# The hand-written order of work between the dense layer and the routed experts is rearranged on all five engines

## The reference

```
h = x @ w_in
g = h where h >= 1, 0 where h <= -1, (h + 1)^2 / 4 between
x = g @ w_out
```

```
logits = x @ w_gate;  e = argmax(logits);  p = softmax(logits)[e]
out[token] = p * (relu(x[token] @ w1[e]) @ w2[e])
```

## Time and profile before

| | |
|---|---|
| median of 3 runs | 822.27 us |
| the profiled execution | 820.93 us |
| its span, first to last instruction | 819.0 us |
| TensorE busy | 763.2 us, 93% |
| VectorE busy | 593.1 us, 72% |
| ScalarE busy | 423.7 us, 52% |
| mean granted TensorE clock | 0.991 |

### The profile page before, as it was taken

The page is one execution under the profiler, slowest core; times in us unless marked ns, Lnnn a source line. Parts: engine busy times, 40 slices in busy tenths (PEclk is TensorE's granted clock), DMA queues, the critical chain, the costliest instruction groups (busy, mean ns, idle before and its releaser), DMA issues. The chain is left out here.

```text
span 819.0 us, 17200 instructions
## 1 busy us (share of the span) xinstructions
PE 763.2 (93%) x5765; PEld 741.7 (91%) x5765; DVE 593.1 (72%) x1006; ACT 423.7 (52%) x649; POOL 319.0 (39%) x297
## 2 busy tenths in 40 slices
PE   2788999999999999999999999979859999999994
PEld 1788999999999999999999999979859999999994
DVE  4653868787878787878878788568667676867850
ACT  3023445454545454545454555655466676767751
POOL 2442544534343445454444544540633323232111
PEclk9999999999999999999999999999988999999998
DMA  6962222222222223232333200542987535545300
GB/s 202 313 168 75 77 92 76 91 75 91 75 91 75 92 81 93 81 96 87 94 86 98 86 24 1 177 123 65 297 303 243 186 108 193 165 153 169 114 21 5
DMA packets 41457, 97.05 MB, mean 119 GB/s; under 512 B 6935, under 2 KB 24481, under 8 KB 39754
## 3 DMA queue, kind: packets, MB, share of 16 engines
q1 hardware_dynamic: 37498, 87.46, 33.7%
q0 software_dynamic: 3920, 9.08, 4.1%
HBM read 105.63 MB, written 9.33 MB: 140 GB/s over the span
## 5 line engine op out<-in xcount | busy, mean ns | idle before, releaser
L545 POOL TENSOR_TENSOR g_t<-u_t,r_t 128x512 f32<-128x512 f32 x96 | 135.8, 1415 | 255.5 <-ACT u_t L695 255.4
L690 ACT ACTIVATE r_t<-bank,neg 128x512 f32<-128x512 f32 x96 | 66.0, 687 | 186.8 <-PE bank L1384 186.8
L1396 PE MATMUL bank<-wo_h,g_h 128*128 128x328 f32 x384 | 127.3, 332 | 2.1 <-DVE g_l L1006 2.1
L1000 DVE TENSOR_SCALAR u_t<-bank 128x512 f32<-128x512 f32 x96 | 66.0, 688 | 75.6 <-ACT r_t L690 52.0
L1396 PE MATMUL bank<-wo_h,g_l 128*128 128x328 f32 x384 | 120.1, 313 | 0.0
L1396 PE MATMUL bank<-wo_l,g_h 128*128 128x328 f32 x384 | 120.1, 313 | 0.0
L627 POOL DMA_INDIRECT out_x<-ob,idx_tok x31 | 38.2, 1234 | 155.0 <-ACT ob L765 150.7
L695 ACT ACTIVATE u_t<-u_t,half 128x512 f32<-128x512 f32 x96 | 69.4, 723 | 40.9 <-DVE u_t L1000 39.7
L936 DVE TENSOR_TENSOR_SCAN W<-W,cst 128x512 f32<-128x512 f32 x48 | 83.4, 1740 | 4.9 <-DMA W<-decays 4.9
L1517 PE MATMUL bank<-w_h,h_h 128*128 128x320 f32 x248 | 78.4, 316 | 2.6 <-DVE w_l L1061 1.5
L1384 PE MATMUL bank<-xT_h,wi_h 128*128 (+1 forms) x384 | 78.8, 287 | 1.6 <-issue 1.6
(11 more groups left out here) (231 smaller groups left out, 1953.3 us busy)
## 6 DMA issues: line engine op xcount, KB each, us to landing
raw<-in_w SPq DMA_DIRECT2D x12, 1280.0 KB
W<-decays SPq DMA_DIRECT2D x24, 512.0 KB, 5.1
raw<-in_w SPq DMA_DIRECT2D x12, 1024.0 KB
raw2n<-in_w SPq DMA_DIRECT2D x7, 1280.0 KB
raw1n<-in_w SPq DMA_DIRECT2D x7, 1024.0 KB
raw<-in_w SPq DMA_DIRECT2D x24, 256.0 KB
qG<-in_q SPq DMA_DIRECT2D x24, 180.0 KB
qT<-in_qt SPq DMA_DIRECT2D x48, 80.0 KB
```

The lines of the kernel that those rows point to most:

```text
L545: pool.tensor_tensor(g_t[p % 2][:, :], u_t[p % 2][:, :], r_t[p % 2][:, :], ALU.add).then_inc(sm["g_done"], 1)
L690: act.activation(r_t[p % 2][:, :], bank_h[p % 2][:, :], ACT.Relu, bias=neg1[:, 0:1]).then_inc(sm["r_done"], 1)
L1000: dve.tensor_scalar(u_t[p % 2][:, :], bank_h[p % 2][:, :], 1.0, -1.0, ALU.min, ALU.max).then_inc(sm["u_done"], 1)
L1396: mm = pe.matmul(bank_acc[tt][:, 0:DL], l[p % 4][:, c], r[:, f, :], start=f == 0 and a == 0, stop=f == NT1 - 1 and a == 2)
```

## The change

No arithmetic is changed. What is changed is order:

- TensorE: `second2(0)` is cut in two, tiles 0 to 3 before `first_wide(1, ...)` and tiles 4 to 7 behind `turn_y(2)` and `turn_experts(2)`. `second2(1)` moves behind `first_wide(2, ...)`, `second2(2)` behind `first2(3)` and `turn_y(4)`, and the loop begins at slot 3.
- ScalarE: `w1_high(1)` and `w1_high(2)` move ahead, `out_gate(0)`, `w2_high(0, 1)`, `w2_high(1)` and `w2_high(2)` move back.
- VectorE: the same for the low parts, and `w2_low(0, 1)` moves behind the operation that writes `rowi`. `w1_low(0)` goes one step later in the last block and `w2_low(0, 0)` goes into `tail`.
- SyncE: `refill(1)` goes ahead of `refill2(0)`; `refill2(1)` goes behind `load_routed2(3)`; from slot 3 on `refill(s)` and `refill2(s - 1)` take turns.
- GpSimd: `gather(2)` moves from `tail` into step 6 of the last block.

```diff
             def last_stores(t):
                 store_x2(t)
+                refill(1)
                 refill2(0)
-                refill(1)
...
             sp.wait_ge(sm["e_listed"], 2)
             load_routed(3)
-            refill2(1)
             refill(2)
             load_routed2(3)
-            refill(3)
-            refill(4)
-            refill2(2)
-            refill2(3)
-            for s in range(5, NS):
+            refill2(1)
+            for s in range(3, NS):
                 refill(s)
                 refill2(s - 1)
...
-                    if not att and p in (4, 5):
+                    if not att and p in (4, 5, 6):
                         gather(p - 4)
...
             h_high(0, 0)
             h_high(0, 1)
-            w2_high(0, 1)
+            w1_high(1, 0)
             h_high(0, 2)
-            w1_high(1, 0)
+            w1_high(1, 1)
             h_high(0, 3)
             y_high(1)
-            w1_high(1, 1)
+            w2_high(0, 1)
+            h_high(1, 0)
+            h_high(1, 1)
+            h_high(1, 2)
+            h_high(1, 3)
+            w1_high(2, 0)
+            y_high(2)
+            w1_high(2, 1)
             act.wait_ge(sm["list_done"], 1)
             out_gate(0)
-            h_high(1, 0)
+            h_high(2, 0)
             w2_high(1, 0)
-            h_high(1, 1)
+            h_high(2, 1)
             w2_high(1, 1)
...
+            h_high(2, 2)
+            h_high(2, 3)
+            w1_high(3, 0)
+            w1_high(3, 1)
+            y_high(3)
             out_gate(1)
-            h_high(2, 0)
...
             w2_high(2, 0)
-            h_high(2, 3)
             w2_high(2, 1)
-            y_high(3)
             w1_high(4, 0)
...
+                        if p in (6, 7):
+                            w1_low(0, p - 6)
 
             def tail(t):
+                w2_low(0, 0)
                 g_low(t, NP1 - 1)
...
             dve.tensor_copy(rowi[:, :], row[:, :]).then_inc(sm["row_ready"], 1)
-            h_low(1, 3)
+            w2_low(0, 1)
+            y_low(2)
+            w1_low(2, 0)
             dve.wait_ge(sm["tab_T"], 3)
...
             dve.tensor_tensor(e_new[:, EARLY:NS], ...).then_inc(sm["e_listed"], 1)
+            w1_low(2, 1)
+            h_low(2, 0)
+            w2_low(1, 0)
+            h_low(2, 1)
             w2_low(1, 1)
-            y_low(2)
-            w1_low(2, 0)
-            w1_low(2, 1)
+            h_low(2, 2)
             dve.wait_ge(sm["tab_T"], 4)
...
                 turn_y(1)
-                second2(0)
+                second2(0, range(0, NT2 // 2))
                 for p in range(4):
                     first_wide(1, p)
+                turn_y(2)
                 turn_experts(2, bank_r[:, 256:384], HALVES)
-                turn_y(2)
-                second2(1)
+                second2(0, range(NT2 // 2, NT2))
+                for p in range(3):
+                    first_wide(2, p)
                 turn_table(2, bank_r[:, 0:128], bank_r[:, 128:256], HALVES)
-                for p in range(4):
-                    first_wide(2, p)
-                second2(2, range(0, 4))
+                first_wide(2, 3)
+                second2(1, range(0, NT2 - 2))
                 turn_y(3)
-                second2(2, range(4, 7))
+                second2(1, range(NT2 - 2, NT2))
                 first2(3)
-                turn_y(4)
-                second2(2, range(7, NT2))
-                turn_h(3)
-                first2(4)
...
-            for s in range(EARLY + 1, NS):
+            for s in range(EARLY, NS):
```

More of the change, by code:

```diff
@@ L609, in tail @@
             def tail(t):
-                gather(2)
                 to_table(t)
@@ L815, in _ @@
             h_high(0, 1)
-            w2_high(0, 1)
+            w1_high(1, 0)
             h_high(0, 2)
-            w1_high(1, 0)
+            w1_high(1, 1)
             h_high(0, 3)
             y_high(1)
-            w1_high(1, 1)
+            w2_high(0, 1)
[6 more added lines that the diff above has]
+            w1_high(2, 1)
             act.wait_ge(sm["list_done"], 1)
             out_gate(0)
-            h_high(1, 0)
+            h_high(2, 0)
             w2_high(1, 0)
-            h_high(1, 1)
+            h_high(2, 1)
             w2_high(1, 1)
[L828 to L832, removed]
-            out_gate(1)
-            h_high(2, 0)
[L835 to L838, removed]
+            h_high(2, 2)
[3 more added lines that the diff above has]
+            y_high(3)
+            out_gate(1)
             w2_high(2, 0)
-            h_high(2, 3)
             w2_high(2, 1)
-            y_high(3)
             w1_high(4, 0)
@@ L1186, in body @@
                             early_tokens()
-                        if p in (5, 6):
-                            w1_low(0, p - 5)
+                        if p in (6, 7):
+                            w1_low(0, p - 6)
             def tail(t):
+                w2_low(0, 0)
                 g_low(t, NP1 - 1)
@@ L1201, in _ @@
             all_blocks(dve, body, ahead, tail, 2)
-            w2_low(0, 0)
             h_low(0, 1)
+            w1_low(1, 0)
+            h_low(0, 2)
             dve.wait_ge(sm["base_ready"], NBLK + 1)
@@ L1209, in _ @@
                                    cst[:, C_K128:C_K128 + AREA].unsqueeze(1).to_broadcast([P, E, AREA]), ALU.is_gt))
-            h_low(0, 2)
-            w2_low(0, 1)
+            h_low(0, 3)
+            y_low(1)
+            w1_low(1, 1)
             then(dve.tensor_reduce(npair[:, :], cmp[:, :, 1:AREA:2], AX.X, ALU.add))
             then(dve.tensor_reduce(neven[:, :], cmp[:, :, 0:AREA:2], AX.X, ALU.add))
-            h_low(0, 3)
-            y_low(1)
-            w1_low(1, 0)
+            h_low(1, 0)
             then(dve.tensor_scalar(shift[:, E:2 * E], npair[:, :], 2.0, None, ALU.mult))
@@ L1220, in _ @@
             then(dve.tensor_tensor_scan(cum[:, :], part[:, :], zer[:, :], 0.0, ALU.add, ALU.add))
-            w1_low(1, 1)
             pairs2 = cum[:, E - 1:E]
@@ L1224, in _ @@
             then(dve.scalar_tensor_tensor(o2[:, :], pairs2, -0.5, cst[:, C_C2:C_C2 + 1], ALU.mult, ALU.add))
+            h_low(1, 1)
             then(dve.tensor_tensor(o1[:, :], o1[:, :], o2[:, :], ALU.min))
@@ L1227, in _ @@
             then(dve.tensor_tensor(o2[:, :], o1[:, :], pairs2, ALU.add))
-            h_low(1, 0)
             then(dve.tensor_tensor(o2[:, :], o2[:, :], cst[:, C_S:C_S + 1], ALU.subtract))
             then(dve.scalar_tensor_tensor(key[:, :], o2[:, :], odd[:, 0:1], cst[:, C_S:C_S + 1], ALU.mult, ALU.add))
+            h_low(1, 2)
             then(dve.tensor_scalar(ind[:, :], cum[:, :], key[:, 0:1], None, ALU.is_le))
@@ L1234, in _ @@
             dve.tensor_copy(eb[:, :], ep[:, 0:1].to_broadcast([P, P])).then_inc(sm["eb_ready"], 1)
-            h_low(1, 1)
-            w2_low(1, 0)
+            h_low(1, 3)
             then(dve.tensor_tensor(drow[:, :], shift[:, 1:2 * E + 1], shift[:, 0:2 * E], ALU.subtract))
@@ L1239, in _ @@
             then(dve.tensor_tensor(drow[:, :], drow[:, :], cst[:, C_DA:C_DA + 2 * E], ALU.add))
-            h_low(1, 2)
             then(dve.tensor_tensor(indr[:, :], ind[:, :], drow[:, :], ALU.mult))
@@ L1262, in _ @@
             dve.tensor_copy(gate_slot[:, 2 * EARLY:HALVES], bank_r[:, 128 + 2 * EARLY:128 + HALVES]).then_inc(sm["list_done"], 1)
-            h_low(2, 0)
+            h_low(2, 3)
             w1_low(3, 0)
-            h_low(2, 1)
             w1_low(3, 1)
-            h_low(2, 2)
+            y_low(3)
             w2_low(2, 0)
-            h_low(2, 3)
             w2_low(2, 1)
-            y_low(3)
             w1_low(4, 0)
```

## The result

The kernel after takes 829.3 us (median of 4 runs, 828.83 to 830.53) against 822.19 for the kernel before on the same chip (4 runs, 820.93 to 823.06). The ratio is 1.009, 95% interval 1.0073 to 1.0108: slower by 7.1 us. I had forecast 824.3 and a range to 828.2. The sign is right, the size is not, and the range misses it by 1.1.

What follows compares the result with a forecast made beforehand. It took the kernel to be bound by when `w1_low(4)` ends, releasing slot 5's `w1` load: through the new stalls 2.0 us later (600.25 against 598.25). Added to the median, 822.27 + 2.0 = 824.3; range 820.8 to 828.2.

Steps and rivals of the forecast that it cites:

- I take TensorE to reach `first_wide(0, 0)` when it did: Start of the routed stage: VectorE's summed work is unchanged, so no shift, bounds 0.8 us either way.
- I take the whole 2.15: Wait of `first_wide(0, 3)` for `h_low(0, 1)`: vanishes entirely, 2.15 us gained, bounds 1.4 and 2.4.
- Stall A: New TensorE wait before tile 4 of `second2(0)`, for the late `w2_low(0, 1)` on VectorE: 3.8 us.
- The load of `w2` for slot 1: SyncE load waiting for `w2_low(0, 1)`: issued at 569.4, lands at 575.5, holding up ScalarE's `w2_high(1, 0)`.
- Stall B: TensorE wait before `first_wide(2, 3)`, for `h_low(2, 1)` behind the late `w2` of slot 1: 1.2 us.
- Stall C: TensorE wait before `turn_y(3)`, for slot 3's gather landing at 589.45: 3.3 us.
- Rival 1: TensorE's clock falls in stall C, perhaps also A; everything behind moves by 1.8 us: 826.1, chance 0.15.
- So 0 to 3.8, and I take 0: Delay of slot 5's `w1` load from slot 4's `w2` now going out ahead: 0 to 3.8 us, taken as 0.
- rival 2: Slot 5's load stands behind slot 4's `w2`: half of 3.8 us gives 826.2, all gives 828.1; chance 0.15.
- Rivals 3 and 4: Slot 3's gather lands in 2.9 us: 821.0, chance 0.20. An assumed wait isn't on the path: 819, chance 0.08.
- Rival 4: A wait, above all slot 1's `w2` load, isn't on the path; slot 5's load leaves 4 us earlier: 819, chance 0.08.

Runs made afterwards that it cites:

- `a_start`: Kernel after with `gather(2)`, `w1_low(0)` and `w2_low(0, 0)` put back where they were before: 831.06 us, ratio 1.0094 to the kernel before.
- `a_w2low`: Kernel after with `w2_low(0, 1)` moved up on VectorE to right behind `w1_low(1, 1)`: 827.41 us, ratio 1.007 to the kernel before.
- `a_warm`: Kernel after with 30 unused TensorE transposes in place of the wait at tile 4 of `second2(0)`: 829.35 us, ratio 1.0068 to the kernel before.
- `b_gather`: Kernel before with only `gather(2)` moved into step 6 of the last block: 823.64 us, ratio 1.0028 to the kernel before.
- `a_queue`: Kernel after with SyncE's loads in the old order from slot 3 on: 827.66 us, ratio 1.0065 to the kernel before.
- `a_all`: Kernel after with the edits of `a_start`, `a_queue` and `a_w2low` together: 826.41 us, ratio 1.0049 to the kernel before.
- `a_gather`: Kernel after with only `gather(2)` put back in GpSimd's tail: 830.55 us, ratio 1.0094 to the kernel before.
- `a_list`: `a_all` with `turn_table(2)` and the two copies ending the list moved earlier: 821.84 us, ratio 0.9981 to the kernel before.

## Why the prediction was wrong, step by step

The chain was the right one, link by link: the late `w2_low(0, 1)`, the list's end, slot 3's gather, `w1_low(4)`, the load of slot 5, one long wait. `first_wide(4, 2)` was to be 2.0 us later and was 9.73 later. The missing 7.7 us, counted in the profiled executions:

| link | predicted | measured | added there |
|---|---|---|---|
| ready for the last-but-one dense `second` | 536.20 | 536.77 | 0.6 |
| tile 4 of `second2(0)` begins | 567.95 | 571.61 | 3.1 |
| gather of slot 3 issued | 582.15 | 585.82 | 0 |
| `w1_low(4)` ends | 600.25 | 604.62 | 0.7 |
| load for slot 5 issued | 601.81 | 606.18 | 0 |
| it lands | 609.91 | 617.65 | 3.4 |
| `first_wide(4, 2)` | 616.8 | 624.54 | 0 |

- **"I take TensorE to reach `first_wide(0, 0)` when it did. The bounds are 0.8 us either way": this is the first term that failed, by 3.1 us.** It was +2.9, not 0, far outside its bounds. Of this 1.8 are waits: those of the last two dense steps grew from 2.1 to 1.05 + 2.85 = 3.9, since pieces of GpSimd's work ran at half their speed beside the moved weight splits and the last `g_t` came late. I had summed VectorE's work and left out what it does to its neighbour. The other 1.1 is the clock, which fell behind the 2.85 us wait and made the dense step's 12 matmuls slower; the step behind them lost 0.2 more. The next term, "I take the whole 2.15", was right. That is 2.9 + 0.2 - 2.15 = +0.9 where I had counted -2.15, and the difference is the 3.1. `a_start` shows the same from the other side: without the three moves tile 4 is reached 0.6 us sooner, not 2.15 later.
- **Stall A** was to be 3.8 and was 3.87. `a_w2low`, which has no such stall, shows that VectorE's order makes it.
- **The load of `w2` for slot 1** went out 1.54 us behind `w2_low(0, 1)`, as predicted (1.53). **Stall B** (1.2) did not come, because TensorE was slowed by then: the four tiles took 5.13 us at the fallen clock and not 3.52. In `a_warm`, with the clock held, it is there with 0.68. From tile 4 to the gather's issue it took 14.21 us, predicted 14.20, and that is luck. I had ScalarE wait for `w2` of slot 1, 6.1 us after its issue. In the chain of after it waits for TensorE, behind the slow tiles, and `a_warm` shows the load landing 5.68 us after its issue. One error of 0.4 made up for the other of 0.5.
- **Stall C** was to be 3.3 and was 3.52. The landing of 7.79 against 7.3 is most of the 0.7; the clock's fall behind it is in the rest.
- **Rival 1 was true, and in more places than I gave it.** It put the fall into stall C, perhaps A. The clock fell at both and at the wait at the start. I had weighed two gaps without a fall, 2.15 and 1.9 us, against one with a fall after 2.8, and called 3.3 "barely longer". By lengths alone it was evidence for the fall, though `b_gather`'s 3.08 us without one shows that length does not settle it. What a fall cost depends on when it came and whether TensorE was on the path: at the start 1.25, in A 0.5 (13.72 from tile 4 to the gather's issue in `a_warm`, 14.21 in after), in C 0.6 against `a_queue`. The 1.8 that I gave for C is right where the fall lies within the wait: 13.77 against 11.96 in `a_w2low`.
- **"So 0 to 3.8, and I take 0" is the second term that failed, by 3.35.** The load took 11.47 us, not 8.10. `a_queue` gets 2.1 of that back with the old order, near the half of rival 2 (1.9). But `a_w2low` and `a_warm` get 1.85 and 2.1 back with the new order kept, and `a_all` with both gets no more, 2.0. So the order is one of the things that must be there for 11.47, and rival 2 is not shown as I wrote it. I dismissed it for `w2`'s lead of 3.4 us, and that was really 3.26. But a lead in the issue is not one in bytes, as two windows of after show: 123 and 266 GB/s, so at most 0.8 MB of all traffic went in these 4 us, where `w2` alone has 1.31. The other 1.2 stands in all of these runs, and its cause is open.

```profile
602.00:604.00 2.00, 2.00 (x16) 2.00 (x15) 2.00 (x2) 2.00 (x3) 1.49 (x2) 1.00 0.54 123
604.00:606.00 2.00, 2.00 (x16) 2.00 (x15) 2.00 (x3) 2.00 (x5) 0.00 (x0) 1.00 0.83 266
```

- **Rivals 3 and 4** are out: the gather landed after 7.79. Rival 4's doubt was right in one place, since the load of `w2` for slot 1 was not what ended last, but that won nothing.

Rival 2 at its half (1.9), rival 1 (1.8) and the start's own bound (0.8) come to 824.3 + 4.5 = 828.8. I had priced each as an alternative to the forecast and never added them up, although nothing kept them from coming together. That this sum comes near 829.3 is luck in part, since rival 1's 1.8 belongs to stall C, where the fall cost 0.6. The range was too narrow for that reason, and because the start's bounds took in only VectorE's order.

**What stays open.** The load for slot 5 took 11.1 to 11.7 us in the kernel after, `a_gather` and `a_start`, but 9.4 and 9.6 in `a_warm` and `a_w2low`, with the same order on the queue and nearly the same distance between the issues (3.26, 3.15 and 3.25), and 9.3 to 9.5 in `a_queue`, `a_all` and `a_list` with the old order. From the issue of slot 4's `w2` to the landing the DMA engines moved 4.46 and 4.45 MB in the kernel after and `a_start` (14.73 us at 303 GB/s, 14.98 at 297), and 4.17 and 3.98 MB in `a_w2low` and `a_warm` (12.87 at 324, 12.50 at 318). So there was more traffic and it went slower. What the extra 0.3 to 0.5 MB were, and why the rate was lower, was not tried. Also, 9.2 were added to the stretch in the profiled executions and 7.1 to the medians. Before's profiled execution was 1.3 faster than its median and after's 1.6 slower, which is 2.8 of the 9.9 between them; the medians' own stretches weren't profiled.

## What to carry to other kernels

An operation that moves beside another engine's work can slow that work: look in the trace for pairs that already overlap and compare their durations with quiet ones, before you price the move at nothing. Where all weights pass through one raw buffer, the chain that counts is release, issue, landing, split: find the last thing that holds the release back (here the end of the list, worth 4.6 us of the stretch in one move, 1.8 of them through the clock), and don't expect an earlier issue to land earlier if the DMA engines are full. And add up the rivals that can hold together before you close the range.

## What the runs showed of the hardware

- GpSimd beside VectorE's splits of weights: a gather's instruction took 2.4 to 2.6 us instead of 0.95 to 1.0, an addition of 128x512 took 2.57 instead of 1.29, and the split of `w2` itself 2.56 instead of 1.48. It is not there each time: a gather's instruction that began together with a split took 0.96, and the halves of `w1`'s split beside it kept their 1.74 to 1.79.
- The granted clock fell within a wait of 3.87 us and some 0.5 and 1.4 us behind waits of 2.85 and 3.52. It stayed at 2.4 GHz behind waits of 2.80 (`a_queue`) and 3.08 us (`b_gather`). 30 short transposes in the wait of 3.87 kept it at 2.4 GHz there, and it fell in the next long one.
- The load of `w1` for slot 5, 1.5 MB, took 8.1 to 13.7 us from issue to landing; the 13.7 are those of the kernel in which it left 4.0 us earlier in the stretch than in the kernel before. A load issued behind it did not change its time (8.28 without, 8.12 with).
